# Column sums at the border of two frames as one-column matmuls onto the rows of the state

## The reference, cut to what matters

```python
# q, k, v, a_re, a_im: batch 2, heads 8, 768 steps, 48 channels
mag = sqrt(a_re**2 + a_im**2)
scale = minimum(mag, 0.999) / (mag + 1e-6)
a_re_n, a_im_n = a_re * scale, a_im * scale
for t in range(S):
    ar, ai = a_re_n[:, :, t, :, None], a_im_n[:, :, t, :, None]
    S_re, S_im = ar * S_re - ai * S_im + kv[t], ar * S_im + ai * S_re     # state: 48 x 48, complex
    y[:, :, t] = q[:, :, t] @ S_re
x = y as (1536 tokens, 384)
x = moe(x)          # top-1 of 8 experts, 384 -> 1024 -> 384
return mlp(x)       # 384 -> 2048 -> 384
```

## Time and profile before

| | |
|---|---|
| runs | 550.78 us median of 3 (550.59 to 551.64) |
| profiled execution | 550.25 us, span 548.3 us, mean granted TensorE clock 0.952 |
| TensorE busy | 469.3 us (86%), 3752 records |
| VectorE busy | 364.2 us (66%), 624 |
| ScalarE busy | 278.4 us (51%), 451 |
| the chain that ended last | PE 73%, DVE 9%, DMA 5%, issue 5%, POOL 3%, ACT 2% |

### The profile page before, as it was taken

How to read it: one execution, slowest core, us unless ns; L and a number is a source line. 1 busy time by engine, 2 the same in 40 slices (tenths; PEclk the granted TensorE clock), 3 DMA queues, 4 the chain that set the end, 5 groups by cost and what they waited for, 6 DMA issues and landing times.

```text
span 548.3 us, 10022 instructions
## 1 busy us (share of the span) xinstructions
PE 469.3 (86%) x3752; PEld 419.0 (76%) x3752; DVE 364.2 (66%) x624; ACT 278.4 (51%) x451; POOL 42.9 (8%) x48
## 2 busy tenths in 40 slices
PE   0529986998997019999999999999999999999995
PEld 0327764876886019999999998898998899989985
DVE  2587798678533407767777776787757877477751
ACT  6998658764436006665666664333324333333212
POOL 2000000000001782000000000000003000020002
PEclk9968999899998558999999999999999999999999
DMA  8970000000000358676666666223224333230001
GB/s 319 422 295 2 1 2 0 3 1 2 2 2 2 140 182 321 182 215 200 203 195 202 183 197 208 85 90 115 87 86 145 90 113 101 73 117 0 1 0 60
DMA packets 22179, 63.69 MB, mean 116 GB/s; under 512 B 2929, under 2 KB 4465, under 8 KB 22129
## 3 DMA queue, kind: packets, MB, share of 16 engines
q1 hardware_dynamic: 20592, 58.27, 32.9%
q0 software_dynamic: 1536, 4.74, 2.3%
HBM read 58.27 MB, written 4.74 MB: 115 GB/s over the span
## 4 chain that ended last, share of the span: by engine, by line
PE 73%; DVE 9%; DMA 5%; issue 5%; POOL 3%; ACT 2%; SPq 2%; DVEq 0%; POOLq 0%; ACTq 0%
PE banks L1146 15%; PE banks L1144 15%; PE banks L1145 15%; PE banks L1154 7%; DMA vv<-v_rows 4%; PE banks L1155 3%; PE banks L992 3%; POOL rows_by_slot L370 3%; PE banks L980 2%; PE banks L983 2%; PE banks L944 2%; PE banks L1011 2%; PE banks L1014 1%; PE banks L1138 1%; PE banks L1040 1%
## 5 line engine op out<-in xcount | busy, mean ns | idle before, releaser
L864 DVE TENSOR_TENSOR w_lo<-raw_early,w_hi 128x768 fp32r<-128x768 f32 x84 | 80.0, 956 | 30.7 <-ACT w_hi L537 29.7
L582 ACT ACTIVATE g_hi<-g_all 128x512 fp32r<-128x512 f32 x48 | 30.3, 632 | 118.7 <-DVE g_all L917 118.7
L537 ACT ACTIVATE w_hi<-raw_early 128x768 fp32r<-128x768 f32 x84 | 70.4, 843 | 33.2 <-PE banks L1155 32.9
L1144 PE MATMUL banks<-w_hi,g_hi 128*128 128x384 f32 x192 | 65.1, 339 | 0.5 <-DVE g_lo L919 0.5
L1146 PE MATMUL banks<-w_hi,g_lo 128*128 128x384 f32 x192 | 65.1, 339 | 0.0
L1145 PE MATMUL banks<-w_lo,g_hi 128*128 128x384 f32 x192 | 64.9, 338 | 0.0
L1154 PE MATMUL banks<-h_hi_lo,w_hi 128*128 128x448 f32 x192 | 64.0, 378 | 0.9 <-DVE h_hi_lo L880 0.7
L919 DVE TENSOR_TENSOR g_lo<-g_all,g_hi 128x512 fp32r<-128x512 f32 x48 | 33.3, 693 | 44.2 <-ACT g_hi L582 44.2
L1144 PE MATMUL banks<-ys_hi,w_hi 128*128 128x512 f32 x144 | 56.1, 389 | 1.2 <-DVE ys_lo L894 1.2
L1146 PE MATMUL banks<-ys_hi,w_lo 128*128 128x512 f32 x144 | 57.1, 397 | 0.0
L1145 PE MATMUL banks<-ys_lo,w_hi 128*128 128x512 f32 x144 | 56.8, 394 | 0.0
(11 more groups left out here) (171 smaller groups left out, 992.1 us busy)
## 6 DMA issues: line engine op xcount, KB each, us to landing
raw_early<-weights SPq DMA_DIRECT2D x84, 384.0 KB, 3.6
raw_late<-weights SPq DMA_DIRECT2D x28, 384.0 KB, 3.5
xq<-q_rows SPq DMA_DIRECT2D x3, 776.0 KB, 16.2
xq<-rows_by_slot SPq DMA_DIRECT2D x12, 194.0 KB, 4.2
kk<-k_rows SPq DMA_DIRECT2D x3, 768.0 KB, 17.6
vv<-v_rows SPq DMA_DIRECT2D x3, 768.0 KB, 18.9
aa<-a_re_rows SPq DMA_DIRECT2D x2, 768.0 KB, 10.4
th<-a_im_rows SPq DMA_DIRECT2D x2, 768.0 KB, 11.7
```

The lines of the kernel that those rows point to most:

```text
L537: A(wh[:, slot, :], raw[slot], ACT.Copy).then_inc(w_hi, 1)
L582: A(gh[:, c % GBUF, :], gg[:, c % GBUF, :], ACT.Copy).then_inc(g_hi, 1)
L864: TT(wl[:, slot, :], raw[slot], wh[:, slot, :].bitcast(F32), ALU.subtract).then_inc(w_lo, 1)
L1144: MM(o, lhsT=whi, rhs=mhi, start=first, stop=False)
```

## The change

`totals_of` no longer multiplies a matrix of ones by the data. For each of the 16 (batch, head) pairs the data itself is the weight operand (`lhsT`), 64 columns of it for rows 0 to 63 and 48 for rows 64 to 111, and one column of ones is the moving operand. Each matmul writes one column of a 112 x 16 piece of bank 0, called `TOT`: row = channel, column = (batch, head). There are two matmuls (rows) for the block before the border, and two more that add the block after it: 64 matmuls in a call where there were 4.

`own_totals`, `hop_sum`, the mask `own` and the tile `totals` are gone. `hop_exp` and `hop_phase` read `TOT` in PSUM directly. Since `TOT` lies in the banks of `CUM`, `L_sums(nxt, 0)` now waits for `hop_exp` (`hop_decay`), and `hop_exp` is issued ahead of the two `exps` on ScalarE. A wait of TensorE for `hop_phi` stands before the last frame, where bank 0 is used for something else.

```diff
-        own = ab("own_row", [DP, D])
-        totals = ab("totals", [DP, BW])
...
+        TOT = bank[0][0:DP, 0:HH]
...
+        HOP_ROWS = (slice(0, SINE), slice(SINE, DP))
...
             def hop_exp(f):
-                act.wait_ge(hop_sums, 2 * f - 1)
-                A(hop[:, 0, :], hop[:, 0, :], ACT.Exp).then_inc(hop_decay, 1)
+                act.wait_ge(totals_made, 2 * f - 1)
+                A(hop[:, 0, :], TOT, ACT.Exp).then_inc(hop_decay, 1)
...
                     if s == 4:
+                        hop_exp(f + 1)
                         exps(f + 1, 0)
                         exps(f + 1, 1)
-                        hop_exp(f + 1)
                         table(ACT.Sin)
...
-            TT(own[:, :], ident[0:DP, 0:D], ident[0:DP, SINE:DP], ALU.add).then_inc(own_ready, 1)
-            dve.wait_ge(own_ready, 1)
...
-            def own_totals(i, f):
-                dve.wait_ge(totals_made, 2 * f + (i - 1))
-                if i == 1:
-                    dve.wait_ge(hop_sums, 2 * f - 1)
-                TT(totals[:, :].rearrange("p (b h d) -> p b h d", b=B, d=D),
-                   CUM[0:DP, :, 0:UW].rearrange("p b (h d) -> p b h d", d=D),
-                   own[:, None, None, :].to_broadcast([DP, B, H, D]), ALU.mult).then_inc(totals_out, 1)
-
-            def hop_sum(i, f):
-                dve.wait_ge(totals_out, 2 * f + (i - 1))
-                dve.tensor_reduce(hop[:, i, :], heads(totals[:, :]), AX_X, ALU.add).then_inc(hop_sums, 1)
-
             def hop_phase(f):
-                dve.wait_ge(hop_sums, 2 * f)
-                reduce_angle(hop[:, 2, :], hop[:, 1, :], hop_steps, 2 * f - 2, hop_phi)
+                dve.wait_ge(totals_made, 2 * f)
+                reduce_angle(hop[:, 2, :], TOT, hop_steps, 2 * f - 2, hop_phi)
...
-                    if s == 4 and nxt is not None:
-                        own_totals(0, nxt)
...
-                    if s == 4:
-                        hop_sum(0, nxt)
...
-                        own_totals(1, nxt)
-                        hop_sum(1, nxt)
                         hop_phase(nxt)
...
             def totals_of(t, f, free, count):
                 pe.wait_ge(free, count)
-                for b in range(B):
-                    MM(CUM[0:DP, b, 0:UW], lhsT=ones[:, 0:DP], rhs=half(t, f - 1, 1, b), start=True, stop=False)
-                    x = MM(CUM[0:DP, b, 0:UW], lhsT=ones[:, 0:DP], rhs=half(t, f, 0, b), start=False, stop=True)
+                for i in range(HH):
+                    a = f * 2 * BW + i * D
+                    for r in HOP_ROWS:
+                        MM(TOT[r, i:i + 1], lhsT=t[:, a - BW:a - BW + r.stop - r.start], rhs=ones[:, 0:1], start=True, stop=False)
+                    for r in HOP_ROWS:
+                        x = MM(TOT[r, i:i + 1], lhsT=t[:, a:a + r.stop - r.start], rhs=ones[:, 0:1],
+                               start=False, stop=True)
                 x.then_inc(totals_made, 1)
...
                     if j == 0:
-                        pe.wait_ge(totals_out, 2 * f - 1)
+                        pe.wait_ge(hop_decay, f)
...
             pe.wait_ge(small_dma, 32)
+            pe.wait_ge(hop_phi, NF - 1)
             attend(NF - 1, None)
```

More of the change, by code:

```diff
@@ L174, in fused_attention_moe_mlp @@
         qkv_here = sem("qkv_here")
-        own_ready = sem("own_ready")
         consts, act_passed = sem("consts"), sem("act_passed")
@@ L186, in fused_attention_moe_mlp @@
             sem("phi_steps"), sem("phi_ready"), sem("phi_abs"), sem("trig_ready"))
-        totals_made, totals_out, hop_sums = sem("totals_made"), sem("totals_out"), sem("hop_sums")
+        totals_made = sem("totals_made")
         hop_decay = sem("hop_decay")
```

## The result

The changed kernel takes 562.29 us (median of 4 runs, 560.54 to 565.35) against 550.68 us; the ratio is 1.022 with a 95% interval of 1.0198 to 1.0243. The forecast was slower, by 2.8 us, in a range of 550.9 to 556.3; it is slower by 11.6 us, outside that range. The profiled execution after took 560.54 us, 10.29 over the one before, and is the fastest of the four.

What follows compares the result with a forecast made beforehand. It took TensorE and ScalarE to bound s = 4 and 5 of each border, then VectorE to s = 7. +3.38 us and -0.61 us gave +2.77, so 553.5 us, range 550.9 to 556.3.

Steps and rivals of the forecast that it cites:

- The sum: Both borders together: +3.38 us at s = 4 and -0.61 us at s = 7, giving +2.77 us.
- T: Length of one call of the new totals on TensorE: forecast 3.40 us, between 2.97 and 3.72.
- the upper end: Slowest pace allowed for the new totals on TensorE: 29.1 ns a record, 3.72 us a call.
- The formula: Change over both borders with the length of a call left open: four times that length minus 10.83 us.
- One column will hardly be faster than eight: Totals on TensorE: weights and issue set the pace, so one-column matmuls were given the eight-column pace, 26.5 ns a record.
- the 48-column row: Matmuls of lines 1011 and 1014 in the old trace: 32 records at 29.1 ns each.
- Rival C: Totals on TensorE: one-column matmuls have a slow pace of their own, 32 to 46 ns; +9.2 us, 560.0; chance 0.08.
- the pair of line 1122: The old trace's only one-column matmul row: two 96-column loads 110 to 158 ns apart, scaled to 32 to 46 ns.
- The wait for `hop_exp`: At s = 4, `L_sums(nxt, 0)` waits for `hop_exp` behind the copy of `y`: 1.72 us over both borders.
- the gain at s = 7: VectorE reaches `hop_phase` 1.84 us sooner per border; TensorE then limits it: -0.61 us first border, 0 second.
- the first pair of VectorE's operations: Removing `own_totals(0)` and `hop_sum(0)` at s = 4 gains 0, since the chain there doesn't pass VectorE.
- `turn_state` as the next thing that `shift_state` waits for: At s = 7, TensorE's `turn_state`, not VectorE, was to be what `shift_state` waits for.

Runs made afterwards that it cites:

- e1: The changed kernel with 48 columns of ones instead of one as moving operand in each of the 64 matmuls of a call: 553.51 us, ratio 1.0055.
- e2: The changed kernel with the old four 384-column matmuls in `totals_of`, each row's own channel not chosen: 549.77 us, ratio 0.9991.
- e3: The changed kernel with only the 32 one-column matmuls of the block after the border in each call: 548.93 us, ratio 0.9977.
- e6: The changed kernel, one-column sums, those over the block before the border issued early, half of `L_sums(nxt, 0)` ahead of the `hop_exp` wait: 548.83 us, ratio 0.9964.
- e8: The kernel before with 64 unread one-column matmuls added on TensorE at s = 2 of the second frame, where it idled: 550.82 us, ratio 1.0.
- e7: The kernel before with 64 unread 48-column matmuls added on TensorE at s = 2 of the second frame, where it idled: 548.76 us, ratio 0.9963.

## Why the prediction was wrong

- **The step that failed.** The sum let everything behind the new matmuls run at the speed of the trace of before. The four calls had 1.00, so I carried 1.00 on, and the price of a call was only its own length T. The runs show in its place: each call takes the granted clock to half, and the transposes, scores, sums and applies behind it pay. That is 6.4 us (after against e1, profiled executions), more than twice the whole change that was forecast. The clock was a term put at nothing without a reason, although the trace of before has a fall of its own behind the idle stretch at 92 to 96 us.
- **The pace was also a little off.** I took 26.5 ns a record from eight-column matmuls and measured 29.2, the upper end: T = 3.74 us. The formula then gives 4 x 3.74 - 10.83 = +4.1, where e1 shows +4.4 in the same stretches. So without the clock the median would have lain inside the range, as e1's 553.51 us does. "One column will hardly be faster than eight" held; the 48-column row, which I kept for the upper end, was the nearer one.
- **Rival C had about the size and not the mechanism.** It forecast 560.0 us from one-column matmuls of a slow pace. Their pace is the ordinary one, 29.2 ns at a clock of 1.00; they slow down their successors. Its evidence, the pair of line 1122 at a granted clock of 0.50, is no evidence for a slow pace; that the pair ran at the low clock I had read as a mere correction. At 0.50 the new matmuls too take 52.5 ns a record.
- **The signs that I had named.** None of the three signs of being wrong came true: the pace is not below 21 ns, VectorE does wait for `turn_state`, and the copy of `y` does hold up `hop_exp`. No sign was about the clock. The distances did tell: the first total to the transposes is 4.30 and 3.89 us (3.5 forecast, 5.1 for C), and, from the start of the totals, `exps` comes 4.45 and 3.10 us later (1.45 and 1.93 forecast) and `wtmp` 1.33 and 1.93 us later (0.61 earlier and level forecast).
- **What was right.** The wait for `hop_exp` (0.58 and 1.06 us measured in e2 against 0.62 and 1.10), the gain at s = 7 and what limits it (1.17 and 0.56 against 1.24 and 0.63), `hop_exp` 0.37 us behind the copy of `y`, the first pair of VectorE's operations worth nothing, and `turn_state` as the next thing that `shift_state` waits for (VectorE idles 1.08 us for it ahead of `wtmp` in the changed kernel, 0.81 in e1).
- **A detail that went otherwise.** In the first border of the changed kernel the sums do not start 0.14 us after the end of `hop_exp` (59.42 + 0.19 = 59.61); L922 starts at 60.02, since the scores at half speed occupy TensorE until then. The wait was hidden by something worse.
- **Open.** Why e3's and e6's late calls kept the clock in the second border; why the low clock behind the idle stretch lasts 3.6 us of work in one kernel and 5.3 in another; and 1 to 2 us in the medians and in the tails, which no stage of the border explains (the changed kernel's median is 11.6 us over before, its profiled execution 10.3).

## What to carry to other kernels

Price a stream of very narrow matmuls twice: by its records (29 ns here at a clock of 1.00, for 1 or 48 columns), and by what it does to the clock of the work behind it. If the weights are what has to be loaded, try more columns behind each: here 48 took no longer than 1 and kept the clock at 1.00, and so did streams of 32. And where TensorE must idle ahead of dense work, put work there that streams columns; 64 otherwise useless matmuls gained 0.37% here.

## What the runs showed of the hardware that I had not expected

- A stretch in which TensorE has 4.00 of 4.00 us busy with one-column matmuls (e8) is followed by a granted clock of 0.57 over the next 4 us, the same as a stretch with 0.17 of 4.00 busy (before). With 48 columns (e7) it is 1.00.
- At a granted clock of 1.00, float32 matmuls of 1 and 48 columns with weights of 64 and 48 columns in turn pass at 29.2 and 29.1 ns a record, and of 8 columns with 64-column weights at 26.5.
- Behind the same 4.01 us of idling TensorE worked at the low clock for 3.62 us in one kernel and 5.27 in another.
- The stretch from `exps` to the totals of `th`, with some 250 records of three engines (204 of TensorE in the first border), has the same length in all ten kernels to 0.01 us (16.36 to 16.37, and 15.75 to 15.76), so that a stage's length tells differences of 0.1 us where the medians of whole runs don't tell 1 us.
